# The opening of a recurrence, experts and MLP kernel, put in another order

## What is computed

```python
def _attn_ref(r, k, v, w, a, b):          # all (4, 8, 768, 40): batch, heads, steps, head dim
    state = np.zeros((B, H, D, D))
    for t in range(S):
        y[:, :, t] = np.einsum('bhd,bhde->bhe', rt, state)
        Sa = np.einsum('bhde,bhe->bhd', state, at)
        state = state * wt[:, :, None, :] - np.einsum('bhd,bhe->bhde', Sa, bt)
        state = state + np.einsum('bhd,bhe->bhde', vt, kt)
    return y

def _moe_ref(x, w_gate, wq, wk, wv, wo):  # x (4, 768, 320), 4 experts of width 64
    for e in range(E):                    # gates: softmax over the top 2 of x @ w_gate
        q, k, v = x @ wq[e], x @ wk[e], x @ wv[e]
        a = causal_softmax(q @ k.T / 8)
        ye = a @ v @ wo[e]
        out += gate[e] * ye               # for the tokens whose top 2 hold e

def _moe2_ref(x, w_in, w_spatial, b_spatial, w_out):
    h = np.maximum(x @ w_in, 0.0)         # 320 -> 1024, split into u and v
    v_n = (v - mean(v)) / sqrt(var(v) + 1e-6)
    v_s = einsum('ts,bsd->btd', w_spatial, v_n) + b_spatial
    return (u * v_s) @ w_out
```

## Time and profile before

| | |
|---|---|
| median of 3 runs | 1078.49 us (1078.14 to 1078.82) |
| profiled execution | 1071.31 us, its span 1069.5 us |
| TensorE matmul busy | 989.7 us, 93% of the span, 15696 instructions |
| VectorE busy | 523.9 us, 49% |
| ScalarE busy | 451.9 us, 42% |
| GpSimd busy | 249.2 us, 23% |
| chain that ended last | TensorE 81%, VectorE 9%, issue 4%, ScalarE 3% |
| mean granted clock of TensorE | 0.984 |

### The profile page before, as it was taken

How to read it: one execution, slowest core, us unless ns; L and a number is a source line. 1 busy time by engine, 2 the same in 40 slices (tenths; PEclk the granted TensorE clock), 3 DMA queues, 4 the chain that set the end, 5 groups by cost and what they waited for, 6 DMA issues and landing times.

```text
span 1069.5 us, 36916 instructions
## 1 busy us (share of the span) xinstructions
PE 989.7 (93%) x15696; PEld 708.6 (66%) x15696; DVE 523.9 (49%) x1443; ACT 451.9 (42%) x1116; POOL 249.2 (23%) x352
## 2 busy tenths in 40 slices
PE   1889999999999999998887999999999999999988
PEld 0478888888888888886644654557545665456555
DVE  5357777777777877755343233322433224331220
ACT  1245555655556565553145243442333423434400
POOL 7334454344444534411000001100011000110011
PEclk9869999999999999999999999999999999999989
DMA  5124434334343433221140100001000000000001
GB/s 154 50 67 119 112 110 124 97 100 151 101 124 101 124 95 111 79 70 48 39 164 1 37 1 1 1 19 56 0 1 1 26 13 0 1 1 26 13 0 37
DMA packets 50645, 63.49 MB, mean 59 GB/s; under 512 B 26545, under 2 KB 36593, under 8 KB 50481
## 3 DMA queue, kind: packets, MB, share of 16 engines
q1 hardware_dynamic: 50480, 61.13, 19.6%
HBM read 53.22 MB, written 7.86 MB: 57 GB/s over the span
## 4 chain that ended last, share of the span: by engine, by line
PE 81%; DVE 9%; issue 4%; ACT 3%; POOL 1%; DMA 1%; SPq 1%; DVEq 0%; POOLq 0%; ACTq 0%
PE banks L1440 13%; PE banks L590 10%; PE banks L635 6%; PE banks L1343 6%; PE banks L1382 5%; PE banks L1362 4%; PE banks L1394 4%; PE banks L1422 4%; PE banks L1409 4%; PE banks L1452 4%; PE banks L820 3%; DVE state_z L1016 3%; PE banks L810 3%; PE banks L1329 3%; PE banks L682 2%
## 5 line engine op out<-in xcount | busy, mean ns | idle before, releaser
L473 ACT ACTIVATE powers_z<-powers,parity 128x256 f32<-128x256 f32 x240 | 108.6, 500 | 168.8 <-DVE powers L891 168.8
L1440 PE MATMUL banks<-w_st,v_n 128*128 128x384 f32 x384 | 151.5, 510 | 4.9 <-issue 4.9
L1223 POOL TENSOR_TENSOR v_st<-v_st,u_t 128x384 f32<-128x384 f32 x32 | 31.9, 998 | 513.5 <-DVE v_st L1589 513.5
L635 PE MATMUL banks<-pq,powers_z 64*64 64x64 f32 (+1 forms) x3072 | 135.0, 226 | 6.1 <-ACT pq L465 3.3
L635 PEld LDWEIGHTS banks<-pq,powers_z 64*64 64x64 f32 x3072 | 114.2, 140 | 11.2 <-ACT powers_z L473 4.1
L1228 ACT ACTIVATE probs_t<-banks 128x512 f32<-128x512 f32 (+1 forms) x96 | 52.0, 542 | 145.4 <-PE banks L1382 145.4
L434 POOL TENSOR_TENSOR state<-state_sum,dc 128x160 f32<-128x160 f32 x92 | 68.6, 746 | 177.7 <-DVE state_sum L1002 177.5
L1440 PEld LDWEIGHTS banks<-w_st,v_n 128*128 128x128 f32 x384 | 65.5, 194 | 44.1 <-issue 19.9
L994 DVE SCALAR_TENSOR_TENSOR vu_tok<-banks,minus,vz_tok 128x80 f32<-128x80 f32 x192 | 48.9, 296 | 81.0 <-PE banks L820 80.9
L1535 DVE CUSTOM_DVE_ANT_0 probs<-banks,hide 128x128 f32<-128x128 f32 (+5 forms) x96 | 56.0, 622 | 66.3 <-PE banks L1362 66.1
L1242 ACT ACTIVATE probs<-probs,neg_max 128x128 f32<-128x128 f32 (+5 forms) x96 | 63.2, 660 | 34.5 <-DVE neg_max L1535 34.5
(11 more groups left out here) (158 smaller groups left out, 1860.1 us busy)
## 6 DMA issues: line engine op xcount, KB each, us to landing
w_ch<-decays_dram SPq DMA_DIRECT2D x48, 160.0 KB
kb_raw<-kb_ch_dram SPq DMA_DIRECT2D x48, 160.0 KB
vz_tok<-vz_tok_dram SPq DMA_DIRECT2D x24, 320.0 KB, 3.5
r_all<-rz_ch_dram SPq DMA_DIRECT2D x48, 160.0 KB
x_dram<-y_tok SPq DMA_DIRECT2D x384, 10.0 KB, 1.9
a_raw<-a_ch_dram SPq DMA_DIRECT2D x48, 80.0 KB
vc_tok<-vc_tok_dram SPq DMA_DIRECT2D x24, 160.0 KB, 3.8
r_all<-r_ch_dram SPq DMA_DIRECT2D x48, 80.0 KB
```

Of the source, the lines that this page charges most:

```text
L473: act.activation(powers_z[:, i, :, j, :], powers[:, i, :, :], ACT.Copy, scale=parity[:, j:j + 1])\
L635: ins = pe.matmul(to[r, k * n:k * n + n], powers_z[r, i, k, :, :].rearrange("p j t -> p (j t)"), right, start=True, stop=True)
L1440: ins = pe.matmul(bank[M_BANK + j % 2][:, 0:TH], v_n[:, i, d * P:d * P + P], w_st[:, i, t], start=(i == 0), stop=(i == BLOCKS - 1))
```

## The change

- The first block goes; `ident` is made among GpSimd's other constants. A one-column tile `nought` is zeroed first.
- `load_fold` stands ahead of `load_first(0)` and `load_first(1)` on SyncE.
- `state_z`, `state` and `vu_tok` are zeroed by ScalarE, with copies of `nought` broadcast, as its first instructions.
- A fold is now a single matmul; 12 in all. The first 6 (groups 0 and 1) stand ahead of TensorE's loop and wait only for their loads. The other 6 stand singly or in a pair behind slots: two at (-2, 0, 0), one each at (-2, 2, 2), (-1, 0, 0), (-1, 1, 0), (-1, 2, 0). Odd groups use bank 0 instead of 7.
- VectorE zeroes the banks, `state_sum` and `g_tok` at slot (-2, 0, 1), behind `first_power(0)`, instead of before its loop.
- Each wait for zeros or constants stands at what reads them first: VectorE's loop needs 4 constants at once, all from u = -2, and the tokens' zeros from u = 0; ScalarE needs all constants and `az_ch`'s zeros; TensorE the constants after its first folds, the rest and the last fold's copy at its first hop. `turn_keys(0)` no longer waits for the folds.

The core of the diff:

```diff
-        FOLD_BANKS = (5, 7)
+        FOLD_BANKS = (5, 0)
...
+        FOLDS = EP * FC * NK
+        folds_after = {(-2, 0, 0): 2, (-2, 2, 2): 1, (-1, 0, 0): 1, (-1, 1, 0): 1, (-1, 2, 0): 1}
+        FIRST_FOLDS = FOLDS - sum(folds_after.values())
...
+            load_fold()
             load_first(0)
             load_first(1)
-            load_fold()
...
-            pool.wait_ge(consts, CONSTS + 2)
-            pool.memset(state_z[:, :], 0.0).then_inc(tokens_zeroed, 1)
-            pool.memset(state[:, :, :, :], 0.0).then_inc(tokens_zeroed, 1)
-            pool.memset(vu_tok[:, :], 0.0).then_inc(tokens_zeroed, 1)
+            pool.wait_ge(consts, CONSTS)
...
-            act.wait_ge(consts, CONSTS + 2)
-            act.wait_ge(zeroed, ZEROED)
+            act.wait_ge(consts, NOUGHT)
+            for tile in (state_z[:, :].rearrange("p u c q x d -> p (u c q x d)"),
+                         state[:, :].rearrange("p u q d -> p (u q d)"),
+                         vu_tok[:, :].rearrange("p u c a x d -> p (u c a x d)")):
+                copy(tile, nought[:, 0:1].to_broadcast([P, tile.shape[1]])).then_inc(tokens_zeroed, 1)
+            for g in range(FIRST_FOLDS // NK):
+                folded(g)
+            act.wait_ge(consts, CONSTS)
+            act.wait_ge(zeroed, AZ_ZEROED)
...
-                for g in range(first_fold(u, 0), first_fold(u, 1)):
-                    folded(g)
+                if u == -1:
+                    folded(2)
...
-                for g in range(first_fold(u, 1), first_fold(u, 2)):
-                    folded(g)
+                if u == -1:
+                    folded(3)
...
-            pe.wait_ge(consts, CONSTS + 2)
-            pe.wait_ge(zeroed, ZEROED)
-            pe.wait_ge(tokens_zeroed, 3)
...
-                if j == 2 and c < 2:
-                    for g in range(first_fold(u, c), first_fold(u, c + 1)):
-                        fold(g)
...
-                        else:
-                            pe.wait_ge(oi_read, EP * FC)
                         turn_keys(v)
...
+                for f in range(folds_upto(u, c, j) - folds_after.get((u, c, j), 0), folds_upto(u, c, j)):
+                    fold(f)
...
+                        else:
+                            pe.wait_ge(oi_read, EP * FC)
+                            pe.wait_ge(zeroed, ZEROED)
+                            pe.wait_ge(tokens_zeroed, TOKENS_ZEROED)
                         pe.wait_ge(akz_read, at(u, akz_read))
...
+            for f in range(FIRST_FOLDS):
+                fold(f)
+            pe.wait_ge(consts, CONSTS)
             for u in range(-2, UNITS + 2):
...
-            dve.memset(az_ch[:, :, :, :], 0.0)
-            for i in (S_BANK, S_BANK + 1):
-                dve.memset(bank[i], 0.0).then_inc(zeroed, 1)
-            dve.memset(state_sum[:, :, :], 0.0).then_inc(zeroed, 1)
-            dve.memset(g_tok[:, :], 0.0).then_inc(zeroed, 1)
-            dve.wait_ge(consts, CONSTS + 2)
-            dve.wait_ge(zeroed, ZEROED)
-            dve.wait_ge(tokens_zeroed, 3)
+            dve.memset(az_ch[:, :, :, :], 0.0).then_inc(zeroed, 1)
+            dve.wait_ge(consts, SCAN_CONSTS)
...
+                if (u, c, j) == (-2, 0, 1):
+                    for i in (S_BANK, S_BANK + 1):
+                        dve.memset(bank[i], 0.0).then_inc(zeroed, 1)
+                    dve.memset(state_sum[:, :, :], 0.0).then_inc(zeroed, 1)
+                    dve.memset(g_tok[:, :], 0.0).then_inc(zeroed, 1)
...
-        with nc.Block() as block:
-            @block.gpsimd
-            def _(pool):
-                pool.memset(ident[:, :], 0.0).then_inc(ready, 1)
```

More of the change, by code:

```diff
@@ L202, in valid, with folds_upto @@
             return 0 <= u < UNITS
-        def first_fold(u, half):
-            return min(max(EP * FC * (2 * (u + 2) + half) // 4, 0), EP * FC)
+        FOLDS = EP * FC * NK
+        folds_after = {(-2, 0, 0): 2, (-2, 2, 2): 1, (-1, 0, 0): 1, (-1, 1, 0): 1, (-1, 2, 0): 1}
+        FIRST_FOLDS = FOLDS - sum(folds_after.values())
+        def folds_upto(u, c, j):
+            return FIRST_FOLDS + sum(n for step, n in folds_after.items() if step <= (u, c, j))
         @block.sync
@@ L352, in _ @@
             pool.memset(parity[:, :], 0.0).then_inc(consts, 1)
-            pool.wait_ge(consts, 6)
-            pool.memset(one_last[:, C - 1:W:C], 1.0).then_inc(consts, 1)
+            pool.wait_ge(consts, 9)
+            pool.affine_select(out=ident[:, :], in_=ident[:, :], compare_op=ALU.not_equal, fill=1.0, base=0,
+                               pattern=[[-1, P]], channel_multiplier=1).then_inc(consts, 1)
             for i, fill in ((0, -1.0), (1, 1.0)):
@@ L604, in grams, with fold @@
                 ins.then_inc(gram_ready, 1)
-            def fold(g):
-                q, f = g // FC, g % FC
-                if g == 0:
+            def fold(f):
+                g, k = f // NK, f % NK
+                q, m = g // FC, (g % FC) * 512
+                if f == 0:
                     pe.wait_ge(fold_loaded, FOLD_LOADS)
-                if g >= 2:
+                if k == 0 and g >= 2:
                     pe.wait_ge(oi_read, g - 1)
-                for k, (o, rows) in enumerate(KT):
-                    ins = pe.matmul(bank[FOLD_BANKS[g % 2]][:, :], w_ot[0:rows, k, q, :],
-                                    w_i[0:rows, k, f * 512:f * 512 + 512], start=(k == 0), stop=(k == NK - 1))
-                ins.then_inc(oi_ready, 1)
+                rows = KT[k][1]
+                ins = pe.matmul(bank[FOLD_BANKS[g % 2]][:, :], w_ot[0:rows, k, q, :], w_i[0:rows, k, m:m + 512],
+                                start=(k == 0), stop=(k == NK - 1))
+                if k == NK - 1:
+                    ins.then_inc(oi_ready, 1)
             def level(u, i, low=0, high=N8):
@@ L984, in chain @@
                 if j == 0:
+                    if (u, c) == (0, 0):
+                        dve.wait_ge(zeroed, ZEROED)
                     dve.wait_ge(g_ready, at(u, g_ready, c + 1))
@@ L1686, in build @@
         shared = Shared(nc, z, stack, weights[1], weights[5])
-        ident = shared.ident
-        ready = stack.enter_context(nc.semaphore("ident_ready"))
-        with nc.Block() as block:
-            @block.gpsimd
-            def _(pool):
-                pool.memset(ident[:, :], 0.0).then_inc(ready, 1)
-                pool.wait_ge(ready, 1)
-                pool.affine_select(out=ident[:, :], in_=ident[:, :], compare_op=ALU.not_equal, fill=1.0, base=0,
-                                   pattern=[[-1, P]], channel_multiplier=1).then_inc(ready, 1)
         with nc.Block() as block:
```

17 lines of the change are left out of this document (13 added, 4 removed).

## The result

The changed kernel takes 1059.09 us (median of 4 runs, 1057.84 to 1060.18) against 1078.32 us (1074.79 to 1078.82) for the kernel before on the same chip: a ratio of 0.9854, 95% interval 0.9826 to 0.9883. The forecast was 1065.1 us, 0.9876 of its base, with a range from 1059.5. The profiled execution takes 1058.97 us, its span is 1057.1.

The account below looks back on a forecast made before the run. TensorE bounds the kernel from 80 us on; in the opening, weight folds stand in the chain of waits with 14.93 us. Gains of 4.1 + 3.7 + 5.6 = 13.4 us off the 1078.49 median give 1065.1 us, range 1059.5 to 1070.5.

Parts of the forecast that it names:

- Start to G: From kernel start to unit 0's first grams: these come at 19.5 instead of 23.58 us, 4.1 us gained.
- The weights ... end at 6.0 to 7.7: Opening transfers: the 1600 KB of weights take 4.3 to 6.0 us, their bytes ending at 6.0 to 7.7 us.
- At no cost: two fold groups: TensorE before the first grams: two fold groups start at about 8, end by 16.2 to 18.4, hidden until 19.5.
- G to H: From unit 0's first grams to unit 1's: 3.7 us gained, bounds 3.1 and 4.4.
- H to L: From unit 1's first grams to level 3 of unit 0: 11.9 us instead of 17.5, 5.6 us gained.
- I take G + 9.2: Unit 1's first grams come 9.2 us after unit 0's first grams, against 12.9 before.
- rebuilt at the mix of clocks seen now: Unit 1's grams to unit 0's level 3, summed at the old trace's clocks, low first: 11.9 us.
- TensorE stays at the high clock: Rival for the opening: single folds fill TensorE's gaps and keep it fast; 18.4 us gained, 1060.1 us; chance 12%.
- Behind L: After level 3 of unit 0: same program but for three waits at the first hop, no gain in the sum.
- Shift the rest by the same amount: After the opening, from 80 us on: TensorE bound, untouched by the change, so the opening's gain carries through whole.
- The weights hold up the unit's loads: Rival for opening transfers: weights drain at 203 GB/s, keys land at 14.6; 10.6 us gained, 1067.9 us; chance 14%.
- Slower: the low clock lasts: Rival beyond the opening: TensorE stays at 0.50, each us losing 0.42; 45 us give 1084 us; chance 7%.

Follow-up runs that it names:

- e5: The changed kernel run and profiled again, unaltered: 1057.27 us, ratio 0.988 to the kernel before.
- e10: The changed kernel with the folds left out, ScalarE filling `w_oi` with zeros instead: 1061.02 us, ratio 0.9899 to the kernel before.
- e12: The changed kernel plus 8 matmuls before the folds, group 1's copy behind `az_ch`, VectorE's zeros later, two matmuls in unit 0's waits: 1055.61 us, 0.985 of before.
- e8: The changed kernel with VectorE's zeros of two banks, `state_sum` and `g_tok` moved from slot (-2,0,1) to (-2,1,2): ratio 0.9879 to the kernel before.
- e1: The changed kernel with its new opening but the folds in their old places, in whole groups of 3: ratio 0.9983 to the kernel before.

## Why the prediction was right, and where it wasn't

- **Start to G** (4.1 forecast, 0.5 in the first profile, 4.2 in e5). The chain was right, and its 19.5 was met by 19.37. Two terms of the sum were mis-sized. "The weights ... end at 6.0 to 7.7", with a landing 1.0 later, came out as a landing at 8.3 to 10.8. And the step "At no cost: two fold groups" took the second group's 3.0 to 5.2 us rightly, but ended "under the wait until 19.5" only for a landing at 8; its own condition, that each us is one on G once the weights land after 11, nearly came true, at 10.8. What stood behind the folds (the copy and `az_ch`, 1.9 us) was left out of that condition. The transfers of the changed kernel:

```profile
GB/s 0 0 0 45 305 174 311 377 332 338 346 320 283 291 113 96 152 74 131 139 172 229 242 242 229 258 250 262 246 254 209 102 33 0 0 0 0 0 0 16
...
r_all<-moe_w_in_dram SPq DMA_DIRECT2D x2, 512.0 KB, 3.8
...
r_all<-moe_w_in_dram SPq DMA_DIRECT2D x1, 256.0 KB, 7.6
```

  The slices show 283 to 377 GB/s from 3 to 7 us, as assumed. After that 74 to 152 remain until 10 while the last weights and the first unit loads share the engines; the 256 KB transfer landed 7.6 us after its issue, the 512 KB ones 3.8. I had read 1.0 us from last byte to landing out of the tail of the earlier trace rows (139 down to 49 from 15.5 on); it was a slow last transfer, and that counts again. Up to 7 us the slices add up to some 1560 KB, the first of the unit's bytes among them: the rate was as forecast, the landing of the last transfer was not.
- The unit loads ran at 243 GB/s with 0.66 of the engines' time over 11 to 13 us. The Trainium skill (DMA: Bandwidth & Descriptors, "Why a DMA increments its semaphore by 16 and not by 1") gives a transfer the largest number of engines, up to 16, that divides the slowest dimension of both its sides, so 10 for 40 rows; 10 of 16 is 0.63, near the 0.66 of this trace.
- **G to H** (3.7 forecast, 4.6 measured, bounds to 4.4; 5.0 in e5). In the first profile the chain of unit 1's `a` with 1.3 us of zeros decided, as in the forecast's upper bound, and single folds stand in the chain of waits with 0.9 us in all. In e5 TensorE decided, as in the forecast: its chain of waits holds single folds of 3.33, 1.05 and 1.52 us, 5.9 together, more than the 5 that the prediction had named as a sign of being wrong. So the folds are hidden in one execution and not in the other, and what was mis-sized in "I take G + 9.2" is the clock: only the first two folds ran slow, the grams, level 0 and the last fold around them fast (0.65, 0.80, 0.64, 0.66 and 1.05 us).
- **H to L** (5.6 forecast, 8.2 measured, 6.7 in e5). The step that failed is "rebuilt at the mix of clocks seen now". The mix doesn't stay when the work is rearranged: levels 1 to 3 all ran at the high clock (1.15 us), in e5 too, as the rival "TensorE stays at the high clock" had it, with 9.6 us for what took 9.23. e10 shows the cause: without matmuls in the gaps the same levels take 1.97, and the stretch 11.94, nearly the forecast's 11.9.
- **Behind L** the forecast had nothing and the rival 2; 2.0 were measured.
- **"Shift the rest by the same amount"** held up to about 3 us: 15.3 at the hop, 12.4 at the end. Unit 0 took back 1.5: from the scan of unit 3 to that of unit 4 it is 20.06 us before and 21.57 after, with a granted clock of 0.67 over 60 to 70 before and 0.53, 0.50 and 0.60 over 50 to 65 after. e12 points at TensorE's pauses there; e8, which took 19.78 us without any change in unit 0, shows that the loss doesn't come in every execution.
- **The sum was met by luck.** Forecast 4.1 + 3.7 + 5.6 = 13.4, measured 0.5 + 4.6 + 8.2 = 13.3 in the first profile: 3.6 us too much in the first stretch against 0.9 and 2.6 too little in the others. In e5 it is 4.2 + 5.0 + 6.7 = 15.9. The 2.0 behind L and the 2.9 lost after the hop, neither of them in the sum, offset each other too.
- **The absolute time.** Subtracting from 1078.49 gave 1065.1; the ratio forecast, 0.9876, lies inside the measured interval, and the profiled executions differ by 12.3 us against 13.4. The medians of the first comparison lie 19.2 us apart. The base was the weak part: over all 47 runs of the kernel before it takes 1065.96 to 1081.94, median 1073.49, and the 4 runs of the first comparison lay near the top. The changed kernel's 8 runs lie at 1054.87 to 1063.37, median 1058.8, so 14.7 us less. That its runs spread less by more than chance isn't settled.
- **The rivals.** "The weights hold up the unit's loads" was half right: the landing was late, and the folds behind it, not the keys, paid. Nothing overtook in one queue: `w_ch` landed 1.1 to 1.8 us behind the last weight in all nine profiles (by the start of VectorE's scan). "Slower: the low clock lasts" did not occur at that size; in the first profile 2.9 us went after the opening. In e1, with the folds left where they were, all of its 3 us and 4 more went; at the largest step TensorE worked 2.73 of 5 us (335 to 340) and its granted clock then read 0.66, and whether the pause or the clock came first isn't shown.

## What to carry to other kernels

Read TensorE's speed off the duration of one repeated matmul, stretch by stretch, and ask of each move which pauses it opens or fills: here matmuls that fill pauses made their neighbours 1.7 times as fast, and leaving them out put the first hop later, not earlier. When a stretch ahead of the loop is filled with "free" work, write down when its inputs land in the worst case and everything that queues behind it on the other engines. Before a gain of about 1% is subtracted from a median, look at how far apart the runs of the same kernel lie. And before a sum that comes out is called right, hold each of its terms against the trace.

## What the hardware showed that I had not expected

- Leaving 12 matmuls out made the next 30 us of TensorE's work slower: levels at 1.97 instead of 1.15 us, the hop 2.3 to 4.9 us later.
- The granted clock column stands at 1.00 over stretches where matmuls take about 1.7 times as long as later (12 fold records in 10.25 against 5.90 us, a level in 1.97 against 1.15), until its first fall in the execution.
- The same six transfers, issued at the same times, land between 8.3 and 10.8 us in different executions. A second queue let the unit's first load land ahead of them (9.93 against 12.6) but no earlier than in one queue (10.09).
- With two matmuls of 1.1 us without use in it, unit 0 took 18.75 us; in the ten other profiles with the new fold places it took 19.8 to 22.5.
